# A fused attention and two-layer-MLP kernel: probabilities transposed in 32x32 squares and moved by DMA, with the softmax two blocks ahead

## The reference, cut to what matters

```python
kv_pool = kv.reshape(B, H // r, r, W // r, r, C).mean(axis=(2, 4))      # r = 4: 768 keys
k = v = kv_pool.reshape(B, -1, C) @ w_sr
s = (q @ k.T) / sqrt(C)
a = exp(s - s.max(-1)); a /= a.sum(-1) + 1e-09
x = a @ v
h = x @ w1_in;  x2 = maximum(0.01 * h, h) @ w1_out                      # 128 -> 2048 -> 128
h = x2 @ w2_in; out = where(h >= 1, h, where(h <= -1, 0, (h + 1)**2 / 4)) @ w2_out
```

## Time and profile before

| | |
|---|---|
| time, median of 3 runs | 1396.45 us (1395.6 to 1396.55) |
| span of the profiled execution | 1394.2 us |
| PE busy | 1368.8 us, 98% |
| DVE busy | 1035.5 us, 74% |
| ACT busy | 950.9 us, 68% |
| POOL busy | 563.7 us, 40% |
| granted TensorE clock | 1.00 |

### The profile page before, as it was taken

How to read it: one execution, slowest core, us unless ns; L and a number is a source line. 1 busy time by engine, 2 the same in 40 slices (tenths; PEclk the granted TensorE clock), 3 DMA queues, 4 the chain that set the end, 5 groups by cost and what they waited for, 6 DMA issues and landing times.

```text
span 1394.2 us, 21088 instructions
## 1 busy us (share of the span) xinstructions
PE 1368.8 (98%) x6320; PEld 1115.3 (80%) x6320; DVE 1035.5 (74%) x1660; ACT 950.9 (68%) x1695; POOL 563.7 (40%) x424
## 2 busy tenths in 40 slices
PE   5999999999999999999999999999999999999997
PEld 4788888888888888888888888888888888888884
DVE  6577777777777777777787777777877777777777
ACT  3676776766767667677676676776766767667665
POOL 2534344334334344343434434344334334344346
PEclk9999999999999999999999999999999999999999
DMA  8000000000000000000000000000000000000000
GB/s 348 16 0 8 9 15 8 8 15 8 8 8 8 15 8 8 15 2 13 8 8 15 8 8 8 8 15 8 8 15 8 8 8 8 15 0 9 8 1 16
DMA packets 9525, 24.44 MB, mean 18 GB/s; under 512 B 1057, under 2 KB 1185, under 8 KB 8865
## 3 DMA queue, kind: packets, MB, share of 16 engines
q1 hardware_dynamic: 9504, 24.19, 4.9%
HBM read 17.89 MB, written 6.29 MB: 17 GB/s over the span
## 4 chain that ended last, share of the span: by engine, by line
PE 95%; DVE 3%; DMA 1%; ACT 0%; issue 0%; SPq 0%; POOL 0%; POOLq 0%
PE sums L487 13%; PE sums L488 13%; PE sums L486 13%; PE hidden L486 13%; PE hidden L488 13%; PE hidden L487 13%; PE attn L488 5%; PE attn L486 5%; PE attn L487 5%; PE attn L507 4%; DVE stage L445 1%; DVE stage L451 1%; DVE probs L411 1%; DMA stage<-kvT 1%; DVE neg_max L377 0%; PE hidden L507 0%
## 5 line engine op out<-in xcount | busy, mean ns | idle before, releaser
L267 POOL TENSOR_TENSOR g_lo<-stage,g_hi 128x512 fp32r<-128x512 f32 x384 | 508.6, 1324 | 790.4 <-ACT g_hi L329 790.3
L458 DVE SCALAR_TENSOR_TENSOR g_lo<-hidden,g_hi 128x512 fp32r<-128x512 f32 x384 | 265.4, 691 | 265.8 <-ACT g_hi L342 264.3
L342 ACT ACTIVATE g_hi<-hidden 128x512 fp32r<-128x512 f32 x384 | 230.0, 599 | 281.1 <-PE hidden L488 271.8
L445 DVE SCALAR_TENSOR_TENSOR stage<-stage 128x512 f32<-128x512 f32 x384 | 270.9, 705 | 23.1 <-ACT stage L351 21.4
L351 ACT ACTIVATE stage<-hidden 128x512 f32<-128x512 f32 x384 | 230.1, 599 | 74.1 <-PE hidden L488 42.6
L451 DVE TENSOR_TENSOR stage<-hidden,stage 128x512 f32<-128x512 f32 x384 | 265.5, 691 | 13.1
L329 ACT ACTIVATE g_hi<-stage 128x512 fp32r<-128x512 f32 x384 | 242.1, 630 | 31.7 <-DVE stage L451 31.6
L486 PE MATMUL sums<-g_hi,w2o_lo 128*128 128x512 f32 x384 | 152.8, 398 | 4.4 <-POOL g_lo L267 2.8
L486 PE MATMUL hidden<-x_hi,w1i_lo 128*128 128x512 f32 x384 | 152.0, 396 | 1.5 <-DVE x_lo L395 1.5
L486 PE MATMUL sums<-g_hi,w1o_lo 128*128 128x512 f32 x384 | 153.3, 399 | 0.0
L488 PE MATMUL sums<-g_lo,w2o_hi 128*128 128x512 f32 x384 | 151.7, 395 | 0.0
(11 more groups left out here) (107 smaller groups left out, 2090.2 us busy)
## 6 DMA issues: line engine op xcount, KB each, us to landing
q_raw<-qT SPq DMA_DIRECT2D x24, 256.0 KB, 2.7
stage<-kvT SPq DMA_DIRECT2D x12, 512.0 KB, 8.8
outT<-stage SPq DMA_DIRECT2D x24, 256.0 KB, 2.0
stage<-w_out SPq DMA_DIRECT2D x2, 1024.0 KB, 14.1
stage<-w_in SPq DMA_DIRECT2D x2, 1024.0 KB, 14.1
stage<-w_inT SPq DMA_DIRECT2D x1, 1024.0 KB, 13.9
probs<-w_sr SPq DMA_DIRECT2D x1, 64.0 KB, 1.9
```

The source lines that it names most:

```text
L267: nc.gpsimd.tensor_tensor(g2_lo[s % RING][:], g2[s % RING], g2_hi[s % RING][:].bitcast(F32), ALU.subtract).then_inc(g2_split, 1)
L342: nc.scalar.activation(g1_hi[s % RING][:], h1[s % HBANKS], ACT.Relu).then_inc(g1_hi_done, 1)
L445: nc.vector.scalar_tensor_tensor(g2[s % RING], g2[s % RING], 1.0, g2[s % RING], ALU.min, ALU.mult).then_inc(bent_done, 1)
L458: nc.vector.scalar_tensor_tensor(g1_lo[s % RING][:], h1[s % HBANKS], 0.0, g1_hi[s % RING][:].bitcast(F32), ALU.max, ALU.subtract).then_inc ...
```

## The change

From block 2 on, the probabilities are transposed without PE. DVE transposes each of the four tiles `probs[t]` (128x768) in one instruction, square by square of 32x32, into `squares`; SP then issues 16 DMAs a block, one for each pair of 32-partition quadrants, each of 98 KB in pieces of 512 bytes, from `squares` to `moved`, where the block stands fully transposed in SBUF. The queries of these blocks are reordered ahead of the kernel so that the result comes in the right order. ACT makes pT_hi(k) from `moved` in slot 8+k, and the subtraction for pT_lo(k) goes from DVE to POOL, behind g2_lo(8+k); `values(k)` stands in slot 9+k behind mlp2_in(9+k). Scores, maximum, exponential and scaling run two blocks ahead (block j+2 in iteration j) and the DVE transposes stand in slots 3, 5, 7, 9. Blocks 0 and 1 are still transposed by PE, and iteration 0 does the softmax of blocks 1 and 2. The sources and targets of the moves lie in memory in which the weights were staged.

```diff
-TRANSPOSE_SLOT = {9 + k: k for k in range(KC)}
-VALUE_SLOT = {10 + k: k for k in range(KC)}
+SPLIT_SLOT = {8 + k: k for k in range(KC)}
+VALUE_SLOT = {9 + k: k for k in range(KC)}
+BLOCK_SLOT = {2 * t + 3: t for t in range(SUB)}
+BY_PE = 2
+SQ = 32
+QUADS = P // SQ
+MOVES = QUADS * QUADS
+FIRST_SCORE = {t: t for t in range(SUB)}
+FIRST_NORMALISE = {t + 1: t for t in range(SUB)}
+FIRST_TRANSPOSE = {5 + i: (2 * i, 2 * i + 1) for i in range(KC // 2)}
+FIRST_VALUE = {6 + i: (2 * i, 2 * i + 1) for i in range(KC // 2)}
+NEXT_SCORE = {7 + 2 * t: t for t in range(SUB)}
+NEXT_EXP = {8 + 2 * t: t for t in range(SUB)}
...
+NEXT_Q_SLOT = 4
...
 # SP
+            def move_squares(a):
+                sp.wait_ge(squares_ready, SUB * (a - BY_PE + 1))
+                sp.wait_ge(pT_split, KC * a)
...
+                for i in range(QUADS):
+                    for j in range(QUADS):
+                        sp.dma_start(moved_by_quad[j * SQ:(j + 1) * SQ, :, i, :],
+                                     squares_by_quad[i * SQ:(i + 1) * SQ, :, j, :]).then_inc(pT_moved, 16)
             def iteration(j, do):
...
+                    load_queries(j + 3)
                 if do.mlp2_end:
                     sp.wait_ge(out_copied, j - 1)
                     sp.dma_start(outT[:, bass.ds((j - 2) * TB, TB)], out_sb).then_inc(out_stored, 16)
+                if do.attend:
+                    move_squares(j + 2)
...
 # POOL, in slot s, behind g2_lo(s)
+                    if do.values and not do.first and s in SPLIT_SLOT:
+                        k = SPLIT_SLOT[s]
+                        pool.wait_ge(pT_hi_done, KC * (j + 1) + k + 1)
+                        nc.gpsimd.tensor_tensor(pT_lo[k][:], pT_raw[k], pT_hi[k][:].bitcast(F32),
+                                                ALU.subtract).then_inc(pT_split, 1)
...
 # ACT, in slot s, behind the ramp(s)
+                        if do.values and s in SPLIT_SLOT:
+                            transposed_hi(j + 1, SPLIT_SLOT[s])
+                        if do.attend and s in EXP_SLOT:
+                            exponentials(j + 2, EXP_SLOT[s])
                     if do.mlp2 and s > 0:
                         g2_high(s - 1)
...
 # DVE
+            def transpose_squares(a, t):
+                dve.wait_ge(probs_ready, SUB * a + t + 1)
...
+                elif t == 0:
+                    dve.wait_ge(pT_moved, 16 * MOVES * (a - BY_PE))
+                nc.vector.transpose(squares_by_tile[:, :, t, :],
+                                    probs[t][:].rearrange("p (b r) -> p b r", r=SQ)).then_inc(squares_ready, 1)
...
 # PE, in slot s, behind mlp2_in(s)
-                    if do.attend and s in TRANSPOSE_SLOT:
-                        transpose(j + 1, TRANSPOSE_SLOT[s])
-                    if do.attend and s < FC - 1 and s in VALUE_SLOT:
-                        values(j + 1, VALUE_SLOT[s])
+                    if do.attend and not do.first and s > 0 and s in SCORE_SLOT:
+                        score(j + 2, SCORE_SLOT[s])
+                    if do.values and not do.first and s in VALUE_SLOT:
+                        values(j + 1, VALUE_SLOT[s], j + 3 if do.attend else NB)
```

More of the change, by code:

```diff
@@ L54 @@
 SPLIT_Q_SLOT = 11
-TRANSPOSE_SLOT = {9 + k: k for k in range(KC)}
-VALUE_SLOT = {10 + k: k for k in range(KC)}
-assert max(VALUE_SLOT) == FC - 1
-Parts = namedtuple("Parts", "mlp1 mlp2 mlp2_end attend split_q")
+SPLIT_SLOT = {8 + k: k for k in range(KC)}
[11 more added lines that the diff above has]
+NEXT_EXP = {8 + 2 * t: t for t in range(SUB)}
+NEXT_NORMALISE = {9 + 2 * t: t for t in range(SUB)}
+NEXT_BLOCK = {min(10 + 2 * t, FC - 1): t for t in range(SUB)}
+NEXT_Q_SLOT = 4
+Parts = namedtuple("Parts", "mlp1 mlp2 mlp2_end values attend split_q first")
 def parts(j):
-    return Parts(j < NB, 1 <= j <= NB, 2 <= j <= NB + 1, j + 1 < NB, j + 2 < NB)
-STEADY = range(2, NB - 2)
+    return Parts(j < NB, 1 <= j <= NB, 2 <= j <= NB + 1, j + 1 < NB, j + 2 < NB, j + 3 < NB, j == 0)
+STEADY = range(2, NB - 3)
 def every_iteration(engine, iteration):
@@ L91, in build @@
         ident = sb("ident", P)
-        stage = [sb(f"stage{k}", FF) for k in range(KC)]
+        stages = sb("stages", KC * FF)
+        stage = [stages[:, k * FF:(k + 1) * FF] for k in range(KC)]
+        squares = stages[:, FF:FF + SUB * KEYS]
+        moved = stages[:, FF + SUB * KEYS:FF + 2 * SUB * KEYS]
+        assert FF + 2 * SUB * KEYS <= (KC - 2) * FF
         W1O_RAW, W1IT_RAW, W1I_RAW, W2I_RAW, W2O_RAW = stage[:5]
@@ L117, in build @@
         out_sb = stage[0][:, 0:TB]
+        squares_by_tile = squares.rearrange("p (b t r) -> p b t r", t=SUB, r=SQ)
+        squares_by_quad = squares.rearrange("p (k q c) -> p k q c", q=QUADS, c=P)
+        moved_by_quad = moved.rearrange("p (k q c) -> p k q c", q=QUADS, c=P)
+        pT_raw = [moved[:, k * TB:(k + 1) * TB] for k in range(KC)]
         hidden = ctx.enter_context(nc.psum_tensor("hidden", [P, 2 * HBANKS * TB], F32))
@@ L282, in exponentials @@
                 act.wait_ge(max_ready, SUB * a + t + 1)
+                if not (isinstance(a, int) and a <= BY_PE):
+                    act.wait_ge(squares_ready, SUB * (a - BY_PE - 1) + t + 1)
                 nc.scalar.activation(probs[t][:], scores_of(a, t), ACT.Exp, bias=neg_max[:, t:t + 1],
@@ L291, in transposed_hi @@
             def transposed_hi(a, k):
[L292 to L293 removed]
+                if by_pe(a):
+                    act.wait_ge(probsT_ready, KC * a + k + 1)
+                else:
+                    act.wait_ge(pT_moved, 16 * MOVES * (a - BY_PE + 1))
+                source = probsT_of(a, k) if by_pe(a) else pT_raw[k]
+                nc.scalar.activation(pT_hi[k][:], source, ACT.Copy).then_inc(pT_hi_done, 1)
             def attended_hi(a):
@@ L342, in iteration @@
                         nc.scalar.activation(g1_hi[s % RING][:], h1[s % HBANKS], ACT.Relu).then_inc(g1_hi_done, 1)
-                    if do.attend and s == FC - 1:
+                    if do.values and s == FC - 1:
                         attended_hi(j + 1)
@@ L460, in iteration @@
                                                        ALU.max, ALU.subtract).then_inc(g1_split, 1)
-                    if do.attend and s == 0:
-                        row_max(j + 1, 0)
-                    if do.attend and s == FC - 1:
+                    if do.first:
+                        if s in FIRST_NORMALISE:
+                            guard_sum(1, FIRST_NORMALISE[s])
+                            invert_sum(1, FIRST_NORMALISE[s])
+                        if s in FIRST_SCORE:
+                            row_max(1, FIRST_SCORE[s])
+                        for k in FIRST_TRANSPOSE.get(s, ()):
+                            transposed_lo(1, k)
+                        if s in NEXT_EXP:
+                            guard_sum(2, NEXT_EXP[s])
+                            invert_sum(2, NEXT_EXP[s])
+                        if s in NEXT_SCORE:
+                            row_max(2, NEXT_SCORE[s])
+                        if s in NEXT_BLOCK:
+                            transpose_squares(2, NEXT_BLOCK[s])
+                    elif do.attend and s == 0:
+                        row_max(j + 2, 0)
+                    if do.values and s == FC - 1:
                         attended_lo(j + 1)
@@ L467, in iteration @@
                         above(s)
[L468 to L474, removed]
+                    if do.attend and not do.first:
+                        if s in EXP_SLOT:
+                            guard_sum(j + 2, EXP_SLOT[s])
+                            invert_sum(j + 2, EXP_SLOT[s])
+                        if s > 0 and s in SCORE_SLOT:
+                            row_max(j + 2, SCORE_SLOT[s])
+                        if s in BLOCK_SLOT:
+                            transpose_squares(j + 2, BLOCK_SLOT[s])
                 if do.mlp1:
@@ L509, in transpose, with values @@
                 last.then_inc(probsT_ready, 1)
-            def values(a, k):
+            def values(a, k, attended):
+                if k == 0 and attended is not None:
+                    pe.wait_ge(exp_done, SUB * attended)
                 pe.wait_ge(pT_split, KC * a + k + 1)
@@ L558, in _ @@
             for k in range(KC):
-                values(0, k)
+                values(0, k, None)
             pe.wait_ge(lin_split, 1)
@@ L613, in iteration @@
                         mlp1_in(s)
-                    if do.attend and s == FC - 1:
-                        values(j + 1, VALUE_SLOT[s])
-                    if do.attend and s == 0:
-                        score(j + 1, 0)
+                    if do.first:
+                        if s in FIRST_SCORE:
+                            score(1, FIRST_SCORE[s])
+                        if s in NEXT_SCORE:
+                            score(2, NEXT_SCORE[s])
+                        for k in FIRST_TRANSPOSE.get(s, ()):
+                            transpose(1, k)
+                        for k in FIRST_VALUE.get(s, ()):
```

(8 more changed lines are left out.)

80 lines of the change are left out of this document (53 added, 27 removed).

## The result

The changed kernel takes 2202.1 us (2201.2 to 2203.7) against 1396.3 of before: 1.577 times as long, 95% interval 1.575 to 1.579. The profiled execution has a span of 2200.7 us, 806.5 more than before.

A forecast was written before the change was run, and what follows sets the result against it. The prediction took TensorE, 98% busy, as the bound: matmul count times spacing. Span 1394.2 - 58 (transposes) + 594 (stalls) + 5 (iteration 0) + 79 (clock) = 2014, with 2.3 for launch and end 2016 us; range 1905 to 2150.

The forecast's parts named there:

- a ring from mlp2_in over ACT and POOL back to values: Slots 9 to 14: values(k) waits for work that starts only after mlp2_in(9+k); 594 us over 22 blocks.
- The predicted stall: PE's wait before values(k): 4.58 us a slot, 4.11 in slot 14, 27.0 us a block.
- The saving: PE's transposes dropped in 22 of 24 blocks: 2.64 us a block, 58 us in all.
- DVE and the moves: Square transposes on DVE cost nothing, at most 83 us; DMA moves take 8 us a block, hidden.
- Iteration 0: PE stalls once at score(2,0) for POOL's split of the third query block: 5 us, bounds 0 and 10.
- the walk of PE to score(2,0): Iteration 0: PE's matmuls, scores and transposes from 40.37 on bring it to score(2,0) at 57.4 us.
- The clock's term: Slower matmuls after PE's rests in 132 stalled slots: 0.6 us a slot, 79 us, between 0 and 176.
- the high end: Stalled slots: all 15 matmuls slow gives 376 us; with return after 3.1 us, 7 slow matmuls give 176.
- rival (a): Stall as computed, but clock low throughout every stalled slot: 376 us instead of 79, 2313 us; chance 0.07.
- (b): Moves late at slot 3 hold DVE and PE: up to 250 us more, about 2141 to 2266; chance 0.07.
- (c): POOL round trip is off PE's path; only the saving and 5 us remain: 1343 us; chance 0.05.
- (d): Change does not do what it says; PE keeps transposing all blocks: 2074 us; chance 0.01.

The follow-up runs named there:

- e1: Changed kernel with pT_lo(k) ahead of g2_lo(7+k) on POOL instead of behind g2_lo(8+k): 1362.7 us, 0.976 of before.
- e6: Changed kernel with e1's order on POOL and values(k) in slot 10+k instead of 9+k: 1353.7 us, 0.970 of before.
- e9: e6 with iteration 0's exponentials, scaling, transposes and values one slot later, and POOL splitting the third query block before the last weight split: 1345.1 us.

## Why the prediction was right or wrong

**Sign and mechanism were right.** The forecast was a ring from mlp2_in over ACT and POOL back to values, 132 times. The predicted stall was 4.58 us a slot, and 27.0 a block. The run with PE kept busy gives it without the clock: 81.0 - 53.69 = 27.3 us a block, or 26.75 without what the fillers add, 589 us in 22 blocks against 594. In the trace PE goes on at 1059.97 instead of 1055.52: 4.45 us, and its second matmul comes 0.34 instead of 0.23 after that, 4.56 in all. That e1 removes all but 0.4 us a block of it by the place of one instruction on POOL shows the cause.

**The saving was right.** 2.64 us a block was predicted, and 56.33 - 53.69 = 2.64 measured. An iteration of before is 56.33 us and not 56, so DVE had 53.69 and not 53.4 us for its work, which changes nothing. By the prediction's own terms an iteration after is 56.33 - 2.64 + 27.0 + 3.6 = 84.3 us; its "near 80" leaves the clock out.

**DVE and the moves were right as costed, at nothing.** The transpose is 0.967 us, near the figure from the maximum (0.947). The figure of the Trainium skill, "VectorE: DVE Perf Modes", The three transpose paths, scaled to six squares, 1.87 us, was nearly twice what one long fp32 instruction took; the measurement decides. The advice of the Trainium skill, "VectorE: DVE Perf Modes", Rules for kernel authors, to leave a full 128x128 transpose to TensorE where PSUM will do, did not hold here either: with the order mended, the squares and moves win 2.64 us a block, because TensorE is the bound (98% busy before) and the other engines have room. The moves took SP 10.45 us to issue instead of 5.6, as one issue, of 192 pieces of 512 bytes, took 0.65 and not 0.35 us (that the pieces are the reason is not shown); it is hidden, since the iterations of e6 are at their 53.69 with it.

**Iteration 0 was too small.** 5 us were predicted and about 13.7 came. The step that failed is the walk of PE to score(2,0) at the spacing of full work, to 57.4. In fact PE waited on the way, for exponentials that stood in the same slot as their scores, and ACT's weight quarters and with them POOL's last split came later: score(2,0) started near 69.8, not 62.7.

```profile
55.51 0.50 PE L588 MATMUL hidden<-x_hi,w1i_lo 128*128 128x512 f32 x1 [2.96 <-DVE g_lo L544]
60.90 1.11 PE L611 MATMUL attn<-ident,probs 128*128 128x128 f32 x4 [4.44 <-ACT probs L343]
69.81 0.50 PE L588 MATMUL hidden<-kT_hi,q_lo 128*128 128x512 f32 x1 [1.46 <-POOL q_lo L287]
```

**The clock's term was wrong, and it is what put the time outside the range.** I had 79 us, between 0 and 176; it is 246 (2202.1 - 1955.7), or some 258 without what the fillers add. Two steps failed. First the choice between the ends: I went by the row of the tail, in which rests of 0.7 us leave the clock alone, though the rests to come were six times as long. The row of the opening, short bursts with rests of 1.43 us and a spacing of 0.42, was nearer in kind and stood for the high end. Second, the high end itself: I took the return after 3.1 us, as in the opening, for the most that a stall could cost inside the range, and left anything above it to rival (a). In the slot from 1050.57 the slow spacing does end 3.1 us after the restart, but in the one from 1059.97 after 4.0 us and in the one from 1069.55 after 4.4 us. Over all 132 slots 7 matmuls are slow in 21 of them, and 10 or more in nearly all the others. With 589, 258 and 13.7 in place of 594, 79 and 5 the sum gives 1394.2 - 58 + 589 + 14 + 258 + 2 = 2199 us, 3 under the measurement.

**The rivals.** (a), the low clock for whole slots, was nearer to the truth than the forecast's share: 258 lies between 176 and 376, and the stalled slots have 7, or more often 10 to 13, slow matmuls of 15. (b), late moves, did not occur: in all the trace shows one wait of DVE for them, 0.4 us. (c), the stall off PE's path, did not occur, but its price of 1343 us is what the mended version, e9, reaches with 1345: the stall is gone there, and iteration 0 costs 4.3 us where (c) had 5. (d) did not occur: PE has 528 instructions fewer, 24 transposes in each of 22 blocks.

## What to carry to other kernels

When work is moved to an engine with room, walk its list in order: what stands ahead of the moved instruction, what that waits for, and whether the waiting ends in something that the consumer issues just before it needs the result. If so, the load of the engine says nothing, and the length of the ring is paid each time; here putting the instruction ahead cut 27 us a block to 0.4, putting the consumer a slot later cut it to 4.3, and both together to nothing. Price a rest of TensorE at its length plus the slow matmuls behind it, and give the second term the whole span from none to all until a row with rests of that length has been seen.

## What the runs showed that I had not expected

A rest of 4.3 us in a slot costs 1.9 us more in slower matmuls, over 40% on top of it; rests of 2.2 us still cost 0.8 in the mean, half of them nothing and half about twice that. Work that nobody reads, put into the rest, made the kernel 246 us faster. The granted clock of the opening is listed as 1.00 although the spacing there is 0.42 us; from then on the list agrees with the spacings (0.67 to 0.84 in the stalled slots, 1.00 with 18 fillers). For the start of a kernel the spacing is the thing to read.
